# Angle signs by ScalarE, Fourier sums of two tiles and products of two blocks per VectorE instruction

## The chip, the cores and the metric

The kernel runs on one core of a Trainium2 chip. A core has TensorE (PE, with PEld for its weight loads), VectorE (DVE), ScalarE (ACT), GpSimd (POOL) and SyncE (SP), which here issues the DMAs. The metric is the device time of one execution in microseconds, taken as the median of several runs.

## The reference

Three stages follow each other: a gated linear recurrence, a Fourier mixing with a channel product, and a token and channel product.

```python
mag = np.sqrt(a_re * a_re + a_im * a_im)
scale = np.minimum(mag, 0.999) / (mag + 1e-06)
a_re_n, a_im_n = (a_re * scale, a_im * scale)
for t in range(S):                       # B, H, S, D = 4, 8, 768, 48
    new_re = ar * S_re - ai * S_im
    new_im = ar * S_im + ai * S_re
    S_re, S_im = (new_re + kv, new_im)   # kv = outer(k_t, v_t)
    y[:, :, t] = np.einsum('bhd,bhde->bhe', q[:, :, t], S_re)
...
X = np.fft.fft(np.fft.fft(x, axis=1), axis=2)
u = x + np.real(X)
un = (u - mean(u)) / np.sqrt(var(u) + 1e-06)
x = u + np.maximum(un @ w_ch1, 0.0) @ w_ch2
...
u = x + token product of x;  out = u + np.maximum(u @ w_ch1, 0.0) @ w_ch2
```

The complex gates are turned into a product of factors and a sum of angles along t: the running magnitude is a scan over logarithms, the running angle a scan over angles in turns. The angle of one gate is arctan of im / (mag + |re|), twice, with its sign and an offset of half a turn changed where re is negative. The queries and keys are multiplied by cosine and sine of the running angle and by the running magnitude, and what is left is attention within blocks of 128 steps and a state carried from block to block.

## The kernel before, in words

`recurrence_and_fourier` (line 41) holds the first two stages up to u; `channel_product` follows twice. Each engine has its instructions written out in its own order, and waits on semaphores with fixed counts.

**Parts and stages.** There are 24 blocks of 128 steps (six for each of four batches), one per iteration m = 0 to 23 of the loop in every engine's program; b, j = divmod(m, 6). The gates are worked on in nine parts: one of one block, one of two, seven of three. `stage_at` (line 72) places six stages of a part, 0 to 5, in the six iterations before its first block. Each part goes through: squares, `squared`, `magnitudes`, `logs` (with the scan of logarithms), `inverses`, `factors`, `ends`, `tangents`, `scaled`, then `arctangents` and `phases` (stage 3: multiplication by the sign, scan of the angles, rounding to the nearest turn), `sines` and `products` of two blocks (stage 4), `products` of the third (stage 5). The first three parts are done ahead of the loop or in its first iterations. Parts whose first block has j = 0 have their stage 3 in an iteration with j = 3, the others in one with j = 0.

**PE in iteration m.** Transposes of block m's keys (`turn_keys`, line 645; not for j = 5), outputs of block m - 1 from `pr` and the state (lines 669 and 671), mixed with the scores of block m (653), the state's update (682), then Fourier work of the batch before: for j = 1 the row of the middle and three width transforms (699, 714), and for j = 2 to 5 one or two of six inverse tiles (`sequence_transform`, lines 728 to 732), which leave in two PSUM banks `f_bank` by turns; last, the transposes of y of block m - 1 (`turn_y`, 690).

**DVE in iteration m.** `advance_state`, `add_transform` for tiles made in the iteration before, `fold_sequence` for j = 1, stages 3, 4 and 5, then `masked` (line 544: scores times mask into `pr`, without which PE can't compute block m's outputs), then stages 0, 1 and 2. DVE works strictly in this order.

**ACT in iteration m.** `arctangents`, `sines`, the copies of the turned keys, squares, magnitudes, inverses, factors, the copy of y to `y_sb`, for j = 1 the copies of the width transforms, and last the copy of turned y (line 360), which waits for the end of PE's iteration.

**SP** writes products of a block to DRAM and reads them back with the axes exchanged (`turn_over`), the same for the end factors (`turn_decay`), and loads the parts. It waits in its own order too; a wait holds back all that stands behind.

`least` (line 112) is the smallest end factor of all parts. Where it is under a floor, a slow exact path is taken behind this function.

Of the kernel before, what the change touches and what calls it, by code (L numbers as in the profile page):

```python
# [11 lines left out]
P = 128  # L12
# [28 lines left out]
def recurrence_and_fourier(nc, lay, c, u_out, w_raw, tok_raw, x_early, w2_early, w1_next, w2_next, steep):  # L41
    with ExitStack() as ctx:
# [31 lines left out]
        GA = 14  # L74
        GV = [12 + 5 * p.chunks for p in parts]
# [24 lines left out]
        dstage = sb("dstage", [P, 2, 3, 3])  # L100
# [11 lines left out]
        least, least_now, at_floor = sb("least", [P, 1]), sb("least_now", [P, 1]), sb("at_floor", [P, 1])  # L112

        bank = [ctx.enter_context(nc.psum_tensor(f"bank{i}", [P, 512], fp32)) for i in range(8)]
        tr_bank, sc_bank, st_bank, y_bank, f_bank = bank[0:2], bank[2:4], bank[4], bank[5], bank[6:8]
# [6 lines left out]
        consts_set, least_step = sem("consts_set"), sem("least_step")  # L122
# [22 lines left out]
        def transformed_at(j):  # L145
            return {2: [0], 3: [1, 2], 4: [3, 4], 5: [5]}.get(j, [])

        def added_at(m):
            b, j = divmod(m, NCH)
            n = b - 2 if j == 0 else b - 1  # L150
            return [(n, i) for i in {3: [0], 4: [1, 2], 5: [3, 4], 0: [5]}.get(j, []) if n >= 0]

        def products_done(p, i):
            return vec0[p.n] + 12 + 3 * p.chunks + 2 * i
# [5 lines left out]
        def _(sp):  # L160
# [44 lines left out]
            def turn_decay(p):  # L205
# [3 lines left out]
                for part in range(2):  # L209
                    sp.dma_start(lay["d_turn"][p.s, part].rearrange("g p t -> p g t"),  # L210
                                 dstage[:, p.s, :, :]).then_inc(d_out[p.s], 16)
# [28 lines left out]
            for m in range(NM):  # L240
# [8 lines left out]
                for n, i in added_at(m - 1):  # L249
                    store_u(n, i)  # L250
                if m % 3 == 1:
# [11 lines left out]
                if m == NM - 3:  # L263
# [6 lines left out]
                    for p in parts[-2:]:  # L270
                        sp.wait_ge(vec_step[p.s], vec0[p.n] + 9)
# [7 lines left out]
            for n, i in added_at(NM - 1):  # L279
                store_u(n, i)  # L280
            store_u(B - 2, 5)
# [7 lines left out]
        def _(act):  # L289
            A = nc.scalar.activation  # L290

            def squares(p):
                s, T = p.s, slice(0, p.T)
                act.wait_ge(gates_in[p.r], 32 * (p.round + 1))
                if p.turn:
                    act.wait_ge(vec_step[s], vec0[p.n - 2] + 9)
# [3 lines left out]
            def magnitudes(p):  # L300
# [27 lines left out]
            def arctangents(p):  # L328
                s, T = p.s, slice(0, p.T)
                act.wait_ge(vec_step[s], vec0[p.n] + 6)  # L330
                A(t3_b[s][:, :, T], t3_b[s][:, :, T], ACT.Arctan).then_inc(act_step[s], 1)

            def sines(p):
                s, T, n = p.s, slice(0, p.T), act0[p.n]
                re, im = re_b[p.r], im_b[p.r]
                act.wait_ge(vec_step[s], vec0[p.n] + 11 + 3 * p.chunks)
                A(re[:, :, T], t3_b[s][:, :, T], ACT.Abs).then_inc(act_step[s], 1)
                A(im[:, :, T], t3_b[s][:, :, T], ACT.Sin, scale=TURN).then_inc(act_step[s], 1)
                act.wait_ge(act_step[s], n + 12)
# [37 lines left out]
            act.wait_ge(consts_set, 2)  # L377
# [1078 lines left out]
```

## Time and profile before

| | us |
|---|---|
| median of 3 runs | 1140.12 |
| the runs | 1132.46, 1140.42, 1140.12 |
| the profiled execution | 1143.03 |
| its span | 1141.3 |
| PE, DVE, ACT busy | 1019.5, 538.2, 341.9 |
| last inverse tile of the recurrence part | ends near 427 |

The profiled execution is 2.9 us above the median, and 1.7 us lie outside its span. The page gives averages over a span of which the recurrence part is the first 430 us; the change lies in it, so windows and timelines of that stretch say more. PE's busy time hides its speed: the same matmul takes twice as long at the lower of its two clocks, and counts as busy for longer.

### The profile page before, as it was taken

The numbers are of one execution on the slowest core, as the hardware profiler recorded it, in microseconds if no ns is written. First come the engines' busy times: TensorE is split into PE (matmuls) and PEld (weight loads), VectorE is DVE, ScalarE is ACT, GpSimd is POOL, SyncE is SP. The second block draws the span as 40 slices with busy tenths as digits, with TensorE's granted clock in tenths as the row PEclk, the third lists the DMA queues.
The fourth block names the chain that finished last, engine by engine and source line by source line (L and its number), as shares of the span: only waits on it lengthen the run. The fifth ranks groups of instructions, "written<-read, shape, count | busy, mean of one in ns | idle before, by whom it ended". The sixth has DMA issues, their size and how long they took to land. (4 is left out here: it accounts for less than half of the span.)

```text
span 1141.3 us, 15470 instructions
## 1 busy us (share of the span) xinstructions
PE 1019.5 (89%) x6034; PEld 992.7 (87%) x6034; DVE 538.2 (47%) x1040; ACT 341.9 (30%) x515; POOL 29.4 (3%) x14
## 2 busy tenths in 40 slices
PE   0269999979979991999999999977999999999998
PEld 0269999969969971999999999977999999999998
DVE  6797786997962338342432332216323322331411
ACT  6654544745620104211122122115221220310310
POOL 0000000000000004000000000004000000000000
PEclk9999997979977985999999999998999999999999
DMA  4569776774657011712102102001000100100000
GB/s 150 167 170 285 211 219 174 232 221 139 195 158 257 29 35 52 263 43 73 38 14 83 41 21 63 21 24 42 15 8 24 46 14 21 41 21 14 7 21 21
DMA packets 96886, 104.77 MB, mean 92 GB/s; under 512 B 13121, under 2 KB 90433, under 8 KB 96834
## 3 DMA queue, kind: packets, MB, share of 16 engines
q1 hardware_dynamic: 96834, 104.07, 29.6%
q8 instruction: 34, 0.56, 0.2%
q14 instruction: 18, 0.15, 0.0%
HBM read 70.93 MB, written 33.11 MB: 91 GB/s over the span
## 5 line engine op out<-in xcount | busy, mean ns | idle before, releaser
L1111 ACT ACTIVATE hh<-mbank 128x384 fp32r<-128x384 f32 x192 | 94.5, 492 | 370.6 <-PE mbank L1295 370.6
L1204 DVE SCALAR_TENSOR_TENSOR hl<-mbank,hh 128x384 fp32r<-128x384 f32 x192 | 107.0, 558 | 200.7 <-ACT hh L1111 200.7
L1293 PE MATMUL mbank<-nTh,w1h 128*128 128x384 f32 x576 | 193.7, 336 | 0.7 <-DVE w1l L1226 0.7
L1294 PE MATMUL mbank<-nTl,w1h 128*128 128x384 f32 x576 | 193.2, 335 | 0.0
L1295 PE MATMUL mbank<-nTh,w1l 128*128 128x384 f32 x576 | 193.1, 335 | 0.0
L1293 PE MATMUL mbank<-w2h,hh 128*128 128x384 f32 x576 | 193.1, 335 | 0.0
L1295 PE MATMUL mbank<-w2h,hl 128*128 128x384 f32 x576 | 192.4, 334 | 0.0
L1294 PE MATMUL mbank<-w2l,hh 128*128 128x384 f32 x576 | 192.4, 334 | 0.0
L1293 PEld LDWEIGHTS mbank<-nTh,w1h 128*128 128x128 f32 x576 | 108.8, 189 | 1.4 <-issue 1.3
L1294 PEld LDWEIGHTS mbank<-nTl,w1h 128*128 128x128 f32 x576 | 108.7, 189 | 0.0
L1295 PEld LDWEIGHTS mbank<-nTh,w1l 128*128 128x128 f32 x576 | 108.7, 189 | 0.0
L1294 PEld LDWEIGHTS mbank<-w2l,hh 128*128 128x128 f32 x576 | 108.2, 188 | 0.0
L1293 PEld LDWEIGHTS mbank<-w2h,hh 128*128 128x128 f32 x576 | 108.2, 188 | 0.0
L1295 PEld LDWEIGHTS mbank<-w2h,hl 128*128 128x128 f32 x576 | 108.1, 188 | 0.0
L653 PE MATMUL bank<-qT,kT 96*128 96x128 f32 x384 | 99.9, 378 | 1.0 <-DMA qT<-q_turn 1.0
L669 PE MATMUL bank<-v_sb,pr 128*128 128x48 f32 x384 | 79.5, 300 | 21.4 <-DVE pr L544 21.4
L669 PEld LDWEIGHTS bank<-v_sb,pr 128*128 128x128 f32 x384 | 76.1, 248 | 22.0 <-DVE pr L544 22.0
L653 PEld LDWEIGHTS bank<-qT,kT 96*128 96x128 f32 x384 | 74.9, 259 | 1.3 <-issue 1.3
L671 PE MATMUL bank<-state,qT 96*128 96x48 f32 x320 | 72.9, 315 | 0.0
L1218 DVE TENSOR_TENSOR out_sb<-mbank,tok_raw 128x384 f32<-128x384 f32 x24 | 13.4, 557 | 125.1 <-PE mbank L1295 125.1
L645 PE MATMUL bank<-ident,kT 96*128 96x96 f32 x160 | 25.2, 297 | 51.1 <-DMA kT<-k_turn 47.9
L645 PEld LDWEIGHTS bank<-ident,kT 96*128 96x128 f32 x160 | 19.8, 172 | 54.9 <-issue 41.3
(149 smaller groups left out, 1308.5 us busy)
## 6 DMA issues: line engine op xcount, KB each, us to landing
kT<-k_turn SPq DMA_DIRECT2D x24, 384.0 KB, 3.5
qT<-q_turn SPq DMA_DIRECT2D x24, 384.0 KB, 4.5
q_turn<-w_raw SPq DMA_DIRECT2D x30, 192.0 KB, 4.5
k_turn<-t SPq DMA_DIRECT2D x24, 192.0 KB, 4.0
k_turn<-w_early SPq DMA_DIRECT2D x24, 192.0 KB, 4.4
u_scratch<-y_sb SPq DMA_DIRECT2D x24, 192.0 KB, 2.7
w_raw<-in_moe_w_ch SPq DMA_DIRECT2D x2, 2304.0 KB, 9.7
x_early<-u_scratch SPq DMA_DIRECT2D x4, 1152.0 KB, 9.8
```

The source lines that it names most:

```text
L645: turned = nc.tensor.transpose(tr_bank[n % 2][:, g * HD2:(g + 1) * HD2], kT[:, r, 4 * half + g, :], ident[0:HD2, 0:HD2])
L653: made = mm(sc_bank[h // 4][:, (h % 4) * P:(h % 4 + 1) * P], kT[:, r, h, :], qT[:, r, h, :], start=True, stop=True)
L669: made = mm(y_bank[:, cols], pr[:, h, :], v_sb[:, p.s, m - p.first, cols], start=True, stop=not later)
L671: made = mm(y_bank[:, cols], qT[:, m % RING, h, :], state[:, n % 3, cols], start=False, stop=True)
L1111: nc.scalar.activation(hh[:, m, :], mm_bank[(g * (KF + TPG) + m) % 2][:, 0:TG], ACT.Relu).then_inc(h_high, 1)
L1204: nc.vector.scalar_tensor_tensor(out=hl[:, m, :], in0=mm_bank[(g * (KF + TPG) + m) % 2][:, 0:TG], scalar=0.0, in1=hh[:, m, :].bitcast(fp32 ...
L1218: nc.vector.tensor_tensor(out_sb[:, i % 2, :], mm_bank[2 + t % 2][:, 0:DM], res[:, i, :], ALU.add).then_inc(out_ready, 1)
L1293: nc.tensor.matmul(out, lh, rh, start=(n == 0), stop=False)
L1294: nc.tensor.matmul(out, lh, rl, start=False, stop=False)
L1295: last = nc.tensor.matmul(out, ll, rh, start=False, stop=(n == len(pairs) - 1))
```

## The change

- The two comparisons of re with zero leave DVE. ACT computes Sign(3 re + 1e-20) into the buffer of im behind each arctangent, and from it the offset 0.25 - 0.25 sign into `t4`. `phases` multiplies by the sign, and its scan reads the offset from `t4`. `t4` had one use (|re|) and has two now; the first part uses its last third (`angles_room`).
- `magnitudes` waits for the last scan of the two parts before, where it waited for the sum with |re| of the part before.
- `products` works on pairs of blocks (`PAIRS`): the first two of a part in one instruction of 768 elements per partition, the third alone.
- The two banks of the inverse tiles are one tensor `f_pair`, and `add_transform` adds two tiles per instruction, except for the last batch. Inverse tiles are made at j = 2 (two), 3 (two), 5 (two), where it was 2 (one), 3 (two), 4 (two), 5 (one), and added at j = 3, 4 and 0 of the next batch.
- Each part has its own room in `dstage`, and the least end factor is found by one reduction behind the loop; `ends` is one copy and no longer waits for `d_out`.
- Counts of semaphores follow.

```diff
-            return {2: [0], 3: [1, 2], 4: [3, 4], 5: [5]}.get(j, [])
+            return {2: [0, 1], 3: [2, 3], 5: [4, 5]}.get(j, [])
...
-            return [(n, i) for i in {3: [0], 4: [1, 2], 5: [3, 4], 0: [5]}.get(j, []) if n >= 0]
+            return [(n, i) for i in {3: [0], 4: [2], 0: [4]}.get(j, []) if n >= 0]
...
-                if p.n:
-                    act.wait_ge(vec_step[1 - s], vec0[p.n - 1] + 3)
-                A(t4[:, :, T], re_b[p.r][:, :, T], ACT.Abs).then_inc(act_step[s], 1)
+                for o in parts[max(p.n - 2, 0):p.n] if p.n > 1 else []:
+                    act.wait_ge(vec_step[o.s], vec0[o.n] + 7 + 3 * o.chunks)
+                A(t4[:, :, angles_room(p)], re_b[p.r][:, :, T], ACT.Abs).then_inc(act_step[s], 1)
...
                 A(t3_b[s][:, :, T], t3_b[s][:, :, T], ACT.Arctan).then_inc(act_step[s], 1)
+                A(im_b[p.r][:, :, T], re_b[p.r][:, :, T], ACT.Sign, scale=3.0,
+                  bias=nearly_zero[:, 0:1]).then_inc(act_step[s], 1)
+                act.wait_ge(act_step[s], act0[p.n] + 12)
+                A(t4[:, :, angles_room(p)], im_b[p.r][:, :, T], ACT.Identity, scale=-0.25,
+                  bias=quarter[:, 0:1]).then_inc(act_step[s], 1)
...
-                if p.turn:
-                    dve.wait_ge(d_out[s], 32 * p.turn)
-                V.tensor_copy(dstage[:, s, :, 0:p.chunks], t2_b[s][:, :, CT - 1:p.T:CT]).then_inc(vec_step[s], 1)
-                dve.wait_ge(vec_step[s], vec0[p.n] + 5)
-                V.tensor_reduce(least_now[:, :], dstage[:, s, :, 0:p.chunks], mybir.AxisListType.XY,
-                                ALU.min).then_inc(least_step, 1)
-                dve.wait_ge(least_step, 2 * p.n + 1)
-                V.tensor_tensor(least[:, :], least[:, :], least_now[:, :], ALU.min).then_inc(least_step, 1)
+                V.tensor_copy(dstage[:, p.n, :, 0:p.chunks], t2_b[s][:, :, CT - 1:p.T:CT]).then_inc(vec_step[s], 1)
...
-                dve.wait_ge(vec_step[s], n + 6)
-                V.tensor_scalar(im[:, :, T], re[:, :, T], 0.0, -2.0 / PI, ALU.is_lt, ALU.mult).then_inc(vec_step[s], 1)
...
-                dve.wait_ge(act_step[s], act0[p.n] + 11)
-                dve.wait_ge(vec_step[s], n + 7)
-                V.scalar_tensor_tensor(out=t3_b[s][:, :, T], in0=im[:, :, T], scalar=1.0 / PI, in1=t3_b[s][:, :, T],
-                                       op0=ALU.add, op1=ALU.mult).then_inc(vec_step[s], 1)
-                dve.wait_ge(vec_step[s], n + 10)
-                V.tensor_scalar(im[:, :, T], re[:, :, T], 0.0, 0.5, ALU.is_lt, ALU.mult).then_inc(vec_step[s], 1)
+                dve.wait_ge(act_step[s], act0[p.n] + 13)
+                V.scalar_tensor_tensor(out=t3_b[s][:, :, T], in0=t3_b[s][:, :, T], scalar=1.0 / PI, in1=im[:, :, T],
+                                       op0=ALU.mult, op1=ALU.mult).then_inc(vec_step[s], 1)
...
-                for i in chunks:
-                    T = slice(i * CT, (i + 1) * CT)
+                for pair in chunks:
+                    i = pair.start
+                    T = slice(i * CT, pair.stop * CT)
...
-            def add_transform(b, i):
-                n = b * NT + i
-                x = y_sb[:, n % YR, :]
-                dve.wait_ge(b_made, n + 1)
-                cc, sn = f_bank[i % 2][:, 0:FH], f_bank[i % 2][:, FH:2 * FH]
+            def add_transform(b, i, tiles):
+                n, halves_done = b * NT + i, len(halves_added) + 1
+                halves_added.append(n)
+                x = y_sb[:, n % YR:n % YR + tiles, :]
+                dve.wait_ge(b_made, n + tiles)
+                f = f_pair[:, i % 2:i % 2 + tiles, :]
+                cc, sn = f[:, :, 0:FH], f[:, :, FH:2 * FH]
...
-            add_transform(B - 2, 5)
-            dve.wait_ge(least_step, 2 * len(parts))
+            add_transform(B - 2, 4, 2)
+            V.tensor_reduce(least[:, :], dstage[:, :, :, :], mybir.AxisListType.XYZ, ALU.min).then_inc(least_found, 1)
+            dve.wait_ge(least_found, 1)
...
                 if b:
-                    pe.wait_ge(b_added, b * NT - 1)
+                    pe.wait_ge(b_added, b * NT)
```

**Where instructions stand now.** On ACT, iteration 15 before (t_1 holds the tangent, then the arctangent of the part):

```order
L360 ACTIVATE yT<-bank 128x3x128 [waits folded,tr_made]
L331 ACTIVATE t_1<-t_1 128x1152 [waits vec_step_1]
L346 ACTIVATE kt<-bank 128x384 [waits tr_made] x2
L297 ACTIVATE x_early<-re 128x1152 [waits vec_step_0,gates_in_2]
L298 ACTIVATE tok_raw<-im 128x1152
L353 ACTIVATE y_sb<-bank 128x384 [waits u_stored_2,y_made]
```

and in the changed kernel, from the same copy of yT (t without a number is `t4`):

```order
L372 ACTIVATE yT<-bank 128x3x128 [waits folded,tr_made]
L338 ACTIVATE t_1<-t_1 128x1152 [waits vec_step_1]
L339 ACTIVATE w_raw<-w_raw,nearly_zero 128x1152
L342 ACTIVATE t<-w_raw,quarter 128x1152 [waits act_step_1]
L358 ACTIVATE kt<-bank 128x384 [waits tr_made] x2
L304 ACTIVATE x_early<-re 128x1152 [waits vec_step_0,gates_in_2]
```

Sign and Identity stand between the arctangent and the copy of the turned keys, kt.

On DVE, iteration 15 before, from `add_transform` to the first scan:

```order
L566 TENSOR_TENSOR y_sb<-y_sb,bank 128x193 [waits b_made]
L567 TENSOR_TENSOR y_sb<-y_sb,bank 128x191
L569 TENSOR_TENSOR y_sb<-y_sb,bank 128x193 [waits b_half]
L570 TENSOR_TENSOR y_sb<-y_sb,bank 128x191
L487 SCALAR_TENSOR_TENSOR t_1<-w_raw,t_1 128x1152 [waits vec_step_1,act_step_1]
L490 TENSOR_SCALAR w_raw<-w_raw 128x1152 [waits vec_step_1]
L499 SCALAR_TENSOR_TENSOR t_1<-t_1,w_raw 128x128 [waits vec_step_1]
```

and now:

```order
L573 TENSOR_TENSOR y_sb<-y_sb,f_pair 128x2x193 [waits b_made]
L574 TENSOR_TENSOR y_sb<-y_sb,f_pair 128x2x191
L576 TENSOR_TENSOR y_sb<-y_sb,f_pair 128x2x193 [waits b_half]
L577 TENSOR_TENSOR y_sb<-y_sb,f_pair 128x2x191
L489 SCALAR_TENSOR_TENSOR t_1<-t_1,w_raw 128x1152 [waits act_step_1]
L501 SCALAR_TENSOR_TENSOR t_1<-t_1,t 128x128 [waits vec_step_1]
```

Four instructions of two tiles stand where four of one tile stood, and the comparison ahead of the scan is gone; what `phases` waits for is ACT's count alone.

On PE, the end of iteration 14 (j = 2) before, from the state's update to `turn_y`:

```order
L682 MATMUL bank<-v_sb,kt 96x48 [waits st_free,tr_free,v_in_1]
L682 MATMUL bank<-v_sb,kt 96x48 x7
L728 MATMUL bank<-a_mid,tok_raw 128x193 [waits a_ready]
L730 MATMUL bank<-a_sb,cs 128x193 x3
L732 MATMUL bank<-a_sb,ss 128x193 x3
L690 MATMUL bank<-ident,y_sb 128x128 [waits tr_free,y_ready]
L690 MATMUL bank<-ident,y_sb 128x128 x2
```

and now (f_pair are the two banks of the inverse tiles):

```order
L691 MATMUL bank<-v_sb,kt 96x48 [waits st_free,tr_free,v_in_1]
L691 MATMUL bank<-v_sb,kt 96x48 x7
L735 MATMUL f_pair<-a_mid,tok_raw 128x193 [waits a_ready]
L737 MATMUL f_pair<-a_sb,cs 128x193 x3
L739 MATMUL f_pair<-a_sb,ss 128x193 x3
L735 MATMUL f_pair<-a_mid,tok_raw 128x193 [waits a_ready]
L737 MATMUL f_pair<-a_sb,cs 128x193 x3
L739 MATMUL f_pair<-a_sb,ss 128x193 x3
L699 MATMUL bank<-ident,y_sb 128x128 [waits tr_free,y_ready]
L699 MATMUL bank<-ident,y_sb 128x128 x2
```

A second inverse tile stands between the first and `turn_y`. In iteration 16 (j = 4) there is none now.

## Rows read from the trace of the kernel before

**Rows 1.** The page, part 1: engine, busy us (share of the span), instructions.

```profile
PE 1019.5 (89%) x6034; PEld 992.7 (87%) x6034; DVE 538.2 (47%) x1040; ACT 341.9 (30%) x515; POOL 29.4 (3%) x14
```

**Rows 2.** What PE waited for, 40 to 450 us: total us, times, longest us.

```profile
PE bank L669 <- DVE pr L544: 21.4, 3, 8.0
```

**Rows 3.** Timeline of PE: start us, us, line, op, operands, [idle before <-releaser].

```profile
68.04 1.51 PE L669 MATMUL bank<-v_sb,pr 128*128 128x48 f32 x6 [6.39 <-DVE pr L544]
...
135.83 1.54 PE L645 MATMUL bank<-ident,kT 96*128 96x96 f32 x8 [1.79 <-DMA kT<-k_turn]
...
239.04 1.51 PE L669 MATMUL bank<-v_sb,pr 128*128 128x48 f32 x6 [7.00 <-DVE pr L544]
...
321.60 1.51 PE L669 MATMUL bank<-v_sb,pr 128*128 128x48 f32 x6 [7.97 <-DVE pr L544]
```

**Rows 4.** Windows of 6 us, PE: length, busy (instructions), granted clock, DMA share, GB/s.

```profile
84.00:90.00 6.00, 6.00 (x30) 1.00 1.03 317
174.00:180.00 6.00, 6.00 (x32) 0.50 0.89 222
240.00:246.00 6.00, 6.00 (x29) 0.50 0.78 285
270.00:276.00 6.00, 6.00 (x59) 1.00 0.19 44
```

**Rows 5.** Timeline of PE: turn_y, which ends an iteration (8; 13, 14, 15; 20, 21).

```profile
186.47 0.85 PE L690 MATMUL bank<-ident,y_sb 128*128 128x128 f32 x3
...
257.53 0.49 PE L690 MATMUL bank<-ident,y_sb 128*128 128x128 f32 x3
...
268.42 0.49 PE L690 MATMUL bank<-ident,y_sb 128*128 128x128 f32 x3
...
281.94 0.49 PE L690 MATMUL bank<-ident,y_sb 128*128 128x128 f32 x3
...
350.67 0.49 PE L690 MATMUL bank<-ident,y_sb 128*128 128x128 f32 x3
...
372.27 0.49 PE L690 MATMUL bank<-ident,y_sb 128*128 128x128 f32 x3
```

**Rows 6.** Timeline of DVE: start of `phases` in iterations 9 and 15, second comparison.

```profile
188.93 1.36 DVE L487 SCALAR_TENSOR_TENSOR t<-im,t 128x1152 f32<-128x1152 f32 x1 [0.94 <-ACT t L331]
...
272.54 1.35 DVE L487 SCALAR_TENSOR_TENSOR t<-w_raw,t 128x1152 f32<-128x1152 f32 x1
...
273.92 0.76 DVE L490 TENSOR_SCALAR w_raw<-w_raw 128x1152 f32<-128x1152 f32 x1
```

**Rows 7.** Timeline of DVE: copy of the end factors, first multiplication of `tangents`.

```profile
304.78 0.16 DVE L459 COPY dstage<-tok_raw 128x9 f32<-128x9 f32 x1
...
305.25 1.35 DVE L470 TENSOR_TENSOR t<-im,t 128x1152 f32<-128x1152 f32 x1
```

**Rows 8.** Timeline of DVE: a 768-element product; then a pair's first, and what follows.

```profile
26.68 0.95 DVE L479 TENSOR_TENSOR w_early<-w_early,x_early 128x768 f32<-128x768 f32 x1
...
154.62 0.56 DVE L515 TENSOR_TENSOR t<-w_early,w_raw 128x384 f32<-128x384 f32 x1
...
158.74 1.28 DVE L544 TENSOR_TENSOR pr<-bank,mask 128x512 f32<-128x512 f32 x2
```

**Rows 9.** Timeline of DVE: first instruction of two tiles' sums, one after the other.

```profile
216.67 0.35 DVE L566 TENSOR_TENSOR y_sb<-y_sb,bank 128x193 f32<-128x193 f32 x1
...
217.84 0.35 DVE L566 TENSOR_TENSOR y_sb<-y_sb,bank 128x193 f32<-128x193 f32 x1
```

**Rows 10.** Timeline of ACT: copy of yT, arctangent, an operation with bias column.

```profile
268.95 0.49 ACT L360 ACTIVATE yT<-bank 128x384 f32<-128x384 f32 x1 [3.05 <-PE bank L690]
...
269.34 1.16 ACT L331 ACTIVATE t<-t 128x1152 f32<-128x1152 f32 x1
...
284.96 1.25 ACT L340 ACTIVATE w_raw<-w_raw,half_pi 128x1152 f32<-128x1152 f32 x1
```

More of the change, by code:

```diff
@@ L72, in recurrence_and_fourier @@
         stage_at = {(p.first - LEAD + k, k): p for p in parts[2:] for k in range(LEAD)}
-        GA = 14
-        GV = [12 + 5 * p.chunks for p in parts]
+        PAIRS = [[range(i, min(i + 2, p.chunks)) for i in range(0, p.chunks, 2)] for p in parts]
+        GA = 16
+        GV = [10 + 3 * p.chunks + 2 * len(PAIRS[p.n]) for p in parts]
         act0 = [GA * p.turn for p in parts]
@@ L150, in added_at, with angles_room @@
             n = b - 2 if j == 0 else b - 1
-            return [(n, i) for i in {3: [0], 4: [1, 2], 5: [3, 4], 0: [5]}.get(j, []) if n >= 0]
+            return [(n, i) for i in {3: [0], 4: [2], 0: [4]}.get(j, []) if n >= 0]
         def products_done(p, i):
-            return vec0[p.n] + 12 + 3 * p.chunks + 2 * i
+            return vec0[p.n] + 10 + 3 * p.chunks + 2 * (i // 2)
+        def angles_room(p):
+            return slice(2 * CT, 3 * CT) if p.n == 0 else slice(0, p.T)
         head_view = lambda ap: ap.rearrange("p (h d) -> p h d", h=H)
@@ L210, in turn_decay @@
                     sp.dma_start(lay["d_turn"][p.s, part].rearrange("g p t -> p g t"),
-                                 dstage[:, p.s, :, :]).then_inc(d_out[p.s], 16)
+                                 dstage[:, p.n, :, :]).then_inc(d_out[p.s], 16)
                 if p.turn:
@@ L250, in _ @@
                     store_u(n, i)
+                    store_u(n, i + 1)
                 if m % 3 == 1:
@@ L278, in _ @@
                     sp.dma_start(w2_early, w2_next.rearrange("(k p) n -> p k n", p=P)).then_inc(w_fetched, 16)
-            for n, i in added_at(NM - 1):
-                store_u(n, i)
-            store_u(B - 2, 5)
+            for i in (4, 5):
+                store_u(B - 2, i)
             for i in range(NT):
@@ L498, in phases @@
                             start = carry[:, 1 - s, g:g + 1] if p.j0 else 0.0
-                        last = V.tensor_tensor_scan(t3_b[s][:, g, T], t3_b[s][:, g, T], im[:, g, T], start, ALU.add, ALU.add)
+                        last = V.tensor_tensor_scan(t3_b[s][:, g, T], t3_b[s][:, g, T], t4[:, g, offset], start, ALU.add, ALU.add)
                     last.then_inc(vec_step[s], 1)
-                    dve.wait_ge(vec_step[s], n + 12 + 3 * i)
+                    dve.wait_ge(vec_step[s], n + 10 + 3 * i)
                     V.tensor_scalar(re[:, :, T], t3_b[s][:, :, T], ROUND, ROUND, ALU.add, ALU.subtract).then_inc(vec_step[s], 1)
-                    dve.wait_ge(vec_step[s], n + 13 + 3 * i)
+                    dve.wait_ge(vec_step[s], n + 11 + 3 * i)
                     V.tensor_tensor(t3_b[s][:, :, T], t3_b[s][:, :, T], re[:, :, T], ALU.subtract).then_inc(vec_step[s], 1)
-                dve.wait_ge(vec_step[s], n + 11 + 3 * p.chunks)
+                dve.wait_ge(vec_step[s], n + 9 + 3 * p.chunks)
                 V.tensor_copy(carry[:, s, :], t3_b[s][:, :, p.T - 1]).then_inc(vec_step[s], 1)
@@ L591, in _ @@
             phases(p1)
-            products(p0, range(1))
+            products(p0, PAIRS[0])
             squared(p2)
-            products(p1, range(2))
+            products(p1, PAIRS[1])
             logs(p2)
@@ L610, in _ @@
                 if (m, 4) in stage_at:
-                    products(stage_at[m, 4], range(2))
+                    products(stage_at[m, 4], PAIRS[stage_at[m, 4].n][0:1])
                 if (m, 5) in stage_at:
-                    products(stage_at[m, 5], [2])
+                    products(stage_at[m, 5], PAIRS[stage_at[m, 5].n][1:2])
                 masked(m)
```

51 lines of the change are left out of this document (28 added, 23 removed).

## The prediction

> **What bounds the kernel now.** The page comes first. TensorE (PE) is busy for most of the span, VectorE (DVE) for about half [rows 1]. The change touches only the recurrence part, which ends with the last inverse tile near 427 us; the 710 us behind it are the two channel products, whose instructions, order and buffers the diff leaves alone. I price those at nothing, and what they cost comes back unchanged.
>
> Inside the recurrence the list of what PE waited for names one DVE instruction, the masked scores `pr` [rows 2], and the timeline of PE puts that wait at three places: the start (output of block 0 at 68.04), block 12 at 239.04 after 7.00 us, block 18 at 321.60 after 7.97 us [rows 3]. The fourth row there is a wait of 1.79 us for a DMA. Between these places PE doesn't wait, so DVE time that is saved there buys nothing unless it brings one of the waits forward.
>
> The second thing is PE's own speed. Two windows of 6 us with PE busy throughout hold 30 and 59 matmuls [rows 4]: the first stretch (up to about 162 us) runs at 1.2 GHz, although its record says 1.00, and most of what comes behind at 2.4. The record reads 0.50 after each long wait for `pr`, and also at 174 to 180 us, where PE was busy without a gap [rows 4]. The fall in iteration 21 (350.67 to 372.27, 21.6 us) costs 8.1 us against the same work in iteration 15 (268.42 to 281.94, 13.5 us) [rows 5].
>
> The Trainium skill (TensorE: Matmul & The Clock Gate, Part 1) says that the clock is low by default, rises with sustained activity and falls after idleness. The falls behind the two waits agree; the busy window at 84 us and the fall at 174 us don't, and the measurement decides. By the page alone the clock would fall at those two waits and nowhere else, the sum below would be the same, and the two cases of a fall fewer or more would have no chance.
>
> **Removed from DVE.** Per part of three blocks: the two comparisons with zero, 0.76 us each and about 0.04 of gap [rows 6], 0.8 and 0.7 net; the reduction and the minimum behind the copy of the end factors, which leave 0.2 of the 0.47 us between the copy and the next row [rows 7], 0.3 saved. The products of a pair: eight instructions take 4.12 us, start to start [rows 8]; four of 768 elements at 0.95 or a little less [rows 8] take 3.6 to 3.8; I take 0.5 saved, between 0.3 and 0.6. Fourier sums: one tile takes 1.17 us [rows 9], two in one call four instructions of 386 elements, priced by the 384-wide rows at 4.12 / 8 = 0.52 each, so 2.0 instead of 2.34. The single reduction at the end and the missing wait on `d_out` in `ends` lie under the outputs of block 23: nothing on the path; if that cover were gone, 0.2 us.
>
> **Added to ScalarE (ACT).** Sign and Identity behind each arctangent, both with a bias column: 1.25 us by the row of that form, against 1.16 without one [rows 10]. Started back to back they lengthen 1.16 us to about 3.5, so +2.35 us per part, and the first DVE instruction of `phases` now waits for the last of them. Behind them on ACT stand the copies of the turned keys, which PE's state update needs 6 us later: covered.
>
> **Moved.** Inverse tile 1 goes from iteration j = 3 to j = 2, tile 3 from 4 to 3, tile 4 from 4 to 5. PE's sum of work is the same. But at j = 3 DVE adds tiles 0 and 1 in one call, ahead of `phases`, so both must be made: one tile more of PE time, about 2.7 us at 2.4 GHz (10.9 us for iteration 14 with one tile, 13.5 for iteration 15 with two [rows 5]), up to twice that at 1.2. The same tile holds back the copy of yT on ACT, and so the arctangent. Past SP's queue nothing new is moved: the two stores of u behind a pair go out together.
>
> **Stretch B, iterations 14 to 18.** Now yT is copied at 268.95 and the arctangent starts at 269.34 [rows 10], ending at 270.5; `phases` starts at 272.54 [rows 6], so ACT had 2.0 us in hand. With the tile and the two operations it starts 2.7 + 2.35 - 2.0 = 3.0 us later. From there to 321.60 [rows 3] DVE has hardly a gap, and its work shrinks by 0.8 + 0.8 (second comparison, twice), 0.7 (first, once), 0.3 (ends), 0.5 (products), and sums 5 x 1.17 - 2 x 2.0 = 1.9: 5.0 in all. The logarithms of iteration 17 have 1 us in hand against ACT now; I charge 0.5 for their wait. Result: 3.0 - 5.0 + 0.5 = **-1.5 us**. PE's own work up to there is the same, less a small wait of 1 us that now comes for block 16 or so, so the long wait ends near 5.5 us, and the clock falls as before.
>
> **Stretch A, iterations 8 to 12.** Here `phases` started at 188.93 [rows 6] with nothing in hand: it was ACT that released it. The second tile is made behind 186.47 [rows 5], where the clock is just rising: 2.9 us. So 2.9 + 2.35 = 5.2 later, 5.0 less work, **+0.2 us** at 239.04 [rows 3].
>
> **Start.** The comparison saved ahead of the first `masked` would bring 68.04 forward by 1.3 us, 0.8 of it that instruction and 0.5 from the first products, which start the chain of DMAs. But PE then meets the wait at 135.83 [rows 3] on a DMA of that chain, which moves only by the 0.5: the rest is given back. **-0.5 us** (0 to -1.3).
>
> **Last batch and end.** In iterations 19 to 23 DVE has no `phases` left and PE doesn't wait: 0. The six single sums at the end keep their form: 0.
>
> **Sum:** -1.5 + 0.2 - 0.5 = -1.8 us. The profiled execution took 1143.0; the median shown is 1140.1, 2.9 lower, so 1138.3, and I say 1138. The unknown costs reach from -5 (no lateness on ACT in B, 1.3 at the start) to +3 (second tile at 1.2 GHz, 0.6 us each of further waits).
>
> **The rivals.**
>
> *All of the saving arrives (0.08).* If the second tile and the two ACT operations came in time, as they would if `phases` were not held at j = 3, both stretches would end 5.0 earlier, the waits would shrink to 2 and 3 us, and PE might keep 2.4 GHz. Taking the slow stretch behind each as two windows of 6 us like 240 to 246 [rows 4], worth half of 12: 1140.1 - 0.5 - 2 x 5.0 - 2 x 6 = 1118. For it: DVE is full there. Against it: 188.93 was released by ACT already.
>
> *One fall of the clock fewer (0.17).* The three times shown are 1132.5, 1140.4, 1140.1; one lies 8 us lower, as much as the fall in iteration 21 costs. The busy stretches in which the clock fell (iterations 8 and 21) look like others in which it didn't (14, 15). With two tiles in a row at j = 2 the light stretch ahead of iteration 21 is broken by more dense work. 1138 - 8 = 1130. That both are missing: 0.03, 1122.
>
> *Slower: the clock falls in the light iteration (0.12).* At j = 4 PE now has no tile at all. The light stretch from the tiles of iteration 21 to those of 23 is 10.9 - 2.7 = 8.2 us plus some 5 of the next (the same work less the keys' transposes, an estimate), 13 to 14 at 2.4 GHz, where a tile stood between before. A fall some 4 us into it, as at 174 us, leaves about 10 us of work at half speed and none of DVE's slack to hide it, because PE is the bound in the last batch: +10, so 1148 when it comes in addition to the others. It decides if the record falls to 0.50 in iteration 22. In iterations 10 and 16 the same fall would mostly eat PE's long wait.
>
> *The change does not do what it says:* if the merged instructions cost as much as those they replace, B loses 2.4 of its 5.0 and A as well, PE's long waits keep their length, and the time is 1140 to 1143, inside the forecast's own spread.
>
> **How the numbers follow.** Forecast 0.60, the rivals as given, both falls missing 0.03 among them. The forecast alone spans 1133 to 1143. 1127 to 1148 takes in the cases of one fall less and one more and leaves out 1118, 1122 and tails, less than 2 in 10. About 1% is what a measurement of this kernel can tell from no change: faster than 1128.7 are the first rival (0.08), both falls missing (0.03) and a third of the 1130 case (0.06): 0.17. Slower than 1151.5 needs two more falls: 0.04. Within: 0.79.
>
> **What would show it.** In the new profile: rows for Sign and Identity near 1.2 us; `phases` of iterations 9 and 15 released by ACT Identity, and starting 4 to 5 and 3 us later; PE waiting 5 to 6.5 us for `pr` of blocks 12 and 18; iteration 10, 16, 22 with no tile near 8.2 us; DVE's total some 25 us lower, ACT's some 20 higher; PE's wait for kT(6) longer by about 0.8. Waits for `pr` under 3 us, or a granted clock that stays at 1.00 behind them, would make it wrong on the fast side; 0.50 in iteration 22 on the slow side.

## The result, and the profile after

| | before | after |
|---|---|---|
| median, us (runs) | 1139.31 (8) | 1147.65 (8) |
| lowest and highest run, us | 1132.46, 1145.16 | 1145.76, 1150.01 |
| ratio, 95% interval | | 1.0091, 1.0061 to 1.0121 |
| profiled execution, us | 1143.03 | 1149.2 |
| last `turn_y` starts at, us | 398.73 | 403.82 |
| profiled execution less that start | 744.3 | 745.4 |

The change made the kernel 0.9% slower; forecast was 0.2% faster. (The ratio is the one on record, with its interval; that of the two medians is 1.0073.) The last row says that all but 1 us of the difference of the two profiled executions lies ahead of the last `turn_y`, so in the recurrence, as the prediction assumed.

The page, busy time by engine (the answer to [rows 1]):

```profile
PE 1021.5 (89%) x6034; PEld 995.0 (87%) x6034; DVE 517.5 (45%) x938; ACT 361.7 (32%) x533; POOL 29.4 (3%) x14
```

DVE lost 20.7 us (25 were forecast), ACT gained 19.8 (20). The 25 were too much by the prediction's own prices: over nine parts and nine pairs of tiles they make about 12 for the comparisons, 4 for the products, 3 for the sums and 3 for the end factors, 22 in all. So the instructions do about what they were priced at. What PE waited for, with total, times and longest, the answer to [rows 2]:

```profile
PE bank L654 <- DMA kT<-k_turn: 49.7, 4, 41.3
PE bank L678 <- DVE pr L547: 14.8, 3, 5.8
PE bank L699 <- ACT y_sb L365: 6.6, 3, 3.0
```

The wait for `pr` shrank from 21.4 us to 14.8. The third line is what changed most: three times, in `turn_y`, PE waits for ScalarE's copy of y, where it was once for 0.6 us before. The timeline of PE at the waits (idle time in brackets), the answer to [rows 3, 5]; L699 is `turn_y`:

```profile
138.83 1.54 PE L654 MATMUL bank<-ident,kT 96*128 96x96 f32 x8 [4.93 <-DMA kT<-k_turn]
187.99 0.49 PE L699 MATMUL bank<-ident,y_sb 128*128 128x128 f32 x3
201.51 0.49 PE L699 MATMUL bank<-ident,y_sb 128*128 128x128 f32 x3
212.83 0.90 PE L699 MATMUL bank<-ident,y_sb 128*128 128x128 f32 x3 [3.00 <-ACT y_sb L365]
231.30 0.49 PE L699 MATMUL bank<-ident,y_sb 128*128 128x128 f32 x3
239.46 0.51 PE L699 MATMUL bank<-ident,y_sb 128*128 128x128 f32 x3
245.61 1.51 PE L678 MATMUL bank<-v_sb,pr 128*128 128x48 f32 x6 [4.51 <-DVE pr L547]
334.45 1.52 PE L678 MATMUL bank<-v_sb,pr 128*128 128x48 f32 x6 [4.51 <-DVE pr L547]
380.01 0.49 PE L699 MATMUL bank<-ident,y_sb 128*128 128x128 f32 x3
388.18 0.51 PE L699 MATMUL bank<-ident,y_sb 128*128 128x128 f32 x3
399.24 0.49 PE L699 MATMUL bank<-ident,y_sb 128*128 128x128 f32 x3
```

From one `turn_y` to the next is one iteration. Iteration 10 (201.51 to 212.83) holds no tile and took 11.3 us, 3.00 of them the wait. Iteration 11 took 18.5; iteration 23, with the same two tiles, took 11.1 (388.18 to 399.24). Windows of PE (PE busy and matmuls, granted clock, DMA share, GB/s) say why:

```profile
204.00:210.00 6.00, 5.84 (x56) 1.00 0.28 91
210.00:216.00 6.00, 3.17 (x16) 0.61 0.82 207
216.00:222.00 6.00, 6.00 (x30) 0.50 0.72 205
...
378.00:384.00 6.00, 5.75 (x48) 1.00 0.47 164
384.00:390.00 6.00, 6.00 (x60) 1.00 0.09 34
```

Behind the new wait the granted clock is 0.50, which is 1.2 GHz, and in iteration 22 (380.01 to 388.18), the same PE work without a wait, it stays at 1.00 (the window 384 to 390 reaches into iteration 23). Why y came late is in ACT's timeline of iteration 10:

```profile
206.55 1.28 ACT L384 ACT_TABLE_LOAD   x1
207.85 1.16 ACT L310 ACTIVATE x_early<-x_early 128x1152 f32<-128x1152 f32 x1
209.04 1.25 ACT L312 ACTIVATE tok_raw<-x_early,ln_eps 128x1152 f32<-128x1152 f32 x1
210.21 1.15 ACT L316 ACTIVATE t<-x_early 128x1152 f32<-128x1152 f32 x1
211.26 1.15 ACT L319 ACTIVATE t<-w_raw 128x1152 f32<-128x1152 f32 x1
212.31 0.47 ACT L365 ACTIVATE y_sb<-bank 128x384 f32<-128x384 f32 x1
```

A table load and the four operations of `magnitudes` stand ahead of the copy of y (L365) in each iteration of stage 1. The kernel before has them in the same order. There the copy was done before PE came to `turn_y`; its two rows:

```profile
211.16 0.47 ACT L353 ACTIVATE y_sb<-bank 128x384 f32<-128x384 f32 x1
213.87 0.49 PE L690 MATMUL bank<-ident,y_sb 128*128 128x128 f32 x3
```

What hid them were the two inverse tiles (5.4 us) that PE made in iteration j = 4 ahead of `turn_y`; the change took both away.

### The profile page after: what moved, and what is told of

The parts are those of the page before. It is cut to its first block and busy times, and to the rows that moved or that the text cites. A ratio compares the mean times of both kernels' runs of the same rounds, so it can differ in the third digit from the quotient of the medians.

```text
span 1147.4 us, 15375 instructions
## 1 busy us (share of the span) xinstructions
PE 1021.5 (89%) x6034; PEld 995.0 (87%) x6034; DVE 517.5 (45%) x938; ACT 361.7 (32%) x533; POOL 29.4 (3%) x14
## 5 line engine op out<-in xcount | busy, mean ns | idle before, releaser
L678 PE MATMUL bank<-v_sb,pr 128*128 128x48 f32 x384 | 81.2, 305 | 14.8 <-DVE pr L547 14.8
L654 PEld LDWEIGHTS bank<-ident,kT 96*128 96x128 f32 x160 | 19.3, 169 | 57.1 <-issue 41.3
```

The lines of the kernel that those rows point to most:

```text
L654: turned = nc.tensor.transpose(tr_bank[n % 2][:, g * HD2:(g + 1) * HD2], kT[:, r, 4 * half + g, :], ident[0:HD2, 0:HD2])
L678: made = mm(y_bank[:, cols], pr[:, h, :], v_sb[:, p.s, m - p.first, cols], start=True, stop=not later)
```

## The experiments

Ratios are to the kernel before on the same chip; the chips of two experiments can differ, so ratios are compared and not medians. The diffs are against the changed kernel unless the text says otherwise, `...` marks what is left out, and changed counts of semaphores are left out everywhere. Iteration lengths are differences of starts of `turn_y`, from one profiled execution of each kernel.

### Which part costs

**e3_single_tiles**: the Fourier part undone.

```diff
-            return {2: [0, 1], 3: [2, 3], 5: [4, 5]}.get(j, [])
+            return {2: [0], 3: [1, 2], 4: [3, 4], 5: [5]}.get(j, [])
...
-                    add_transform(n, i, 2)
+                    add_transform(n, i, 1)
...
```

> The changed kernel with its Fourier part undone: the table of tiles and one tile per DVE instruction as before; signs on ACT, paired products and the single reduction stay. W and L: the falls in 10 and 16 go, the one in iteration 8 or 21 may come back: 1136 to 1142. A: 1146 to 1149.

**e4_signs_dve**: the comparisons back on DVE.

```diff
-                A(im_b[p.r][:, :, T], re_b[p.r][:, :, T], ACT.Sign, ...)
...
-                A(t4[:, :, angles_room(p)], im_b[p.r][:, :, T], ACT.Identity, ...)
...
+                V.tensor_scalar(im[:, :, T], re[:, :, T], 0.0, -2.0 / PI, ALU.is_lt, ALU.mult).then_inc(vec_step[s], 1)
...
+                V.tensor_scalar(im[:, :, T], re[:, :, T], 0.0, 0.5, ALU.is_lt, ALU.mult).then_inc(vec_step[s], 1)
```

> The changed kernel with its signs undone: both comparisons back on DVE, no Sign and Identity on ACT; paired tiles with their new table and paired products stay. W and L: the wait for y_sb and the falls stay, DVE has 1.6 us more work per part: 1146 to 1152. A: the lateness of phases goes, 1137 to 1141.

**e5_fourier_alone**: e4, and the products block by block.

```diff
-        PAIRS = [[range(i, min(i + 2, p.chunks)) for i in range(0, p.chunks, 2)] for p in parts]
+        PAIRS = [[range(i, i + 1) for i in range(p.chunks)] for p in parts]
```

> The kernel before with the new places of the inverse tiles, the sums of two tiles per instruction and the single reduction of the end factors; signs and offset by VectorE and products block by block, as before. Theory (the new places of the tiles carry the loss): ratio to before 1.006 to 1.014, PE waiting near 3 us for y_sb in iterations 10 and 16. Rival (the loss needs the parts together): 0.998 to 1.004.

**e8_two_sums**: tiles made and added at the new places, but by two calls.

```diff
-                    add_transform(n, i, 2)
+                    add_transform(n, i, 1)
+                    add_transform(n, i + 1, 1)
```

> The changed kernel, tiles made and added at the same places, but each pair added by two calls of one tile (eight instructions of 193 or 191 elements in place of four of 386 or 382). Theory (the places carry the loss, not the merged instruction): within 2 us of the changed kernel, ratio to before 1.007 to 1.013, DVE busy some 2 us more. Rival (the merged instruction holds DVE back): ratio 0.998 to 1.003.

| kernel | median, us | ratio, 95% interval |
|---|---|---|
| e3_single_tiles | 1136.18 | 0.9978, 0.9948 to 1.0008 |
| e4_signs_dve | 1148.41 | 1.0119, 1.0070 to 1.0169 |
| e5_fourier_alone | 1143.97 | 1.0091, 1.0054 to 1.0127 |
| e8_two_sums | 1144.45 | 1.0078, 1.0049 to 1.0106 |

Without the Fourier part the loss is gone; alone it is there in full. All four lie with the theory that was put down for them. PE's waits for `y_sb` are three and 6.6 us in sum in e4, e5 and e8, as in the changed kernel, and one of 0.6 us in e3. So it is the place of the tiles and not the merged instruction. Signs on ACT cost nothing that can be seen.

### The wait for y, or the place without a tile

**e1_y_early** moves ACT's copy of y between the two exponentials of the magnitudes, **e7_y_first** ahead of both, in all iterations that have stage 1 (j = 1 and 4).

```diff
                 A(t2_b[s][:, :, T], t1_b[s][:, :, T], ACT.Exp, scale=-0.5, ...)
+                if m_now:
+                    evacuate_y(m_now - 1)
```

> The changed kernel, with one thing moved on ACT: in an iteration with stage 1 (m = 4, 10, 16) the copy of y to y_sb stands between the first and second Exp of magnitudes, not behind |re|. Theory W (wait): at j = 4 PE has no inverse tile, meets turn_y at once and waits 3.0 us for y_sb, which ACT copies behind magnitudes; this idle time makes the clock fall in iterations 10 and 16. Then the wait shrinks to 1 us or less, both falls go, and the time is 1134 to 1140. Theory L (light work): the clock falls because the iteration has no dense matmuls, wait or not. Then the falls stay and the time is 1145 to 1149. Theory A (Sign and Identity make DVE late): 1146 to 1149.

> The changed kernel, with ScalarE's copy of y moved ahead of both exponentials of the magnitudes, right behind their logarithm, so that PE should not wait for y_sb at all in iterations 4, 10 and 16 (0.9 us were left when the copy stood one instruction later). Theory W (the wait drops the clock in iterations 10 and 16): no fall there, ratio to before 0.985 to 0.993. Theory L (the iteration without a tile is too light, whatever the wait): the clock falls in iterations 10 and 16 all the same, ratio 0.998 to 1.004.

**e2_tile_in_4** puts a tile back to j = 4, so that the second pair is added at j = 5.

```diff
-            return {2: [0, 1], 3: [2, 3], 5: [4, 5]}.get(j, [])
+            return {2: [0, 1], 3: [2], 4: [3], 5: [4, 5]}.get(j, [])
```

> The changed kernel, with inverse tile 3 made in iterations with j = 4 and the pair 2, 3 added at j = 5: tiles 0,1 / 2 / 3 / 4,5 for j = 2, 3, 4, 5. Still two tiles per DVE instruction. Theories W and L both expect the wait for y_sb and the falls in iterations 10 and 16 gone: 1134 to 1140. Theory A expects no change: 1146 to 1149.

**e9_filler** fills j = 4 with the matmuls of a tile made for nothing, into the bank that `turn_y` overwrites; the output is the same. **e16_filler_10_16** has it in iterations 10 and 16 alone.

```diff
+                if m >= NCH and (m + 1) % NCH == 4:      # e16: if m + 1 in (10, 16)
+                    out = tr_bank[n % 2]
+                    mm(out[:, 0:FH], alt[:, 0:P], a_mid[:, :], start=True, stop=False)
+                    ...
                 pe.wait_ge(y_ready, m + 1)
```

> The changed kernel, with the matmuls of one inverse tile made once more and for nothing in iterations 10, 16 and 22, ahead of turn_y, into the bank that turn_y then overwrites: 2.7 us of useless PE work where PE waited 3.0 us for y_sb. Theory (the place without a tile costs by the wait and by the clock that falls behind it): the wait becomes 0.3 us, no fall behind it in iterations 10 and 16, 7.4 us each less and 2.7 more in iteration 22: ratio to before 0.996 to 1.001. Rival (the wait only costs its own length): the filler buys nothing, ratio 1.009 to 1.014.

> The changed kernel with the useless tile in iterations 10 and 16 alone. In e9_filler (10, 16 and 22) the last batch took 78.2 us from turn_y of block 17 to that of block 23, with a fall of the clock near 380 us, in the changed kernel 75.5 without one. Theory (it fell because of the filler's place, and 2.7 us of filler there pay nothing): 3 us less than e9_filler, ratio to before 0.993 to 0.997. Rival (a fall comes in the last batch anyway): as e9_filler or above, 0.997 to 1.001.

| kernel | median, us | ratio, 95% interval | wait for y in iterations 10 and 16, us each | iteration 10 / 11, us |
|---|---|---|---|---|
| before | | | none | 13.5 / 8.4 (2 tiles / 1) |
| after | 1147.65 | 1.0091, 1.0061 to 1.0121 | 3.0 | 11.3 / 18.5 (0 / 2) |
| e1_y_early | 1136.93 | 1.0016, 0.9991 to 1.0042 | 0.9 | 9.2 / 19.3 |
| e7_y_first | 1139.01 | 1.0029, 0.9999 to 1.0059 | none | 8.2 / 17.2 |
| e2_tile_in_4 | 1144.05 | 1.0100, 1.0065 to 1.0135 | none | 19.2 / 11.1 |
| e9_filler | 1133.56 | 0.9986, 0.9962 to 1.0010 | 0.3 | 11.3 / 11.1 |
| e16_filler_10_16 | 1129.59 | 0.9945, 0.9924 to 0.9967 | 0.3 | 11.3 / 11.1 |

e9_filler is the clearest: PE does 2.7 us of useless work where it had waited 3.0, iteration 10 takes as long as in the changed kernel, and iteration 11 falls from 18.5 to 11.1 us. Its windows over the same stretch:

```profile
204.00:210.00 6.00, 5.68 (x48) 1.00 0.62 184
210.00:216.00 6.00, 6.00 (x37) 1.00 0.84 235
216.00:222.00 6.00, 5.75 (x53) 1.00 0.93 276
```

Since the useless work takes as long as the wait did, what the filler gains is the clock: e16_filler_10_16 is 1.5% under the changed kernel by ratio (0.9945 to 1.0091, 17 us). In the profiled executions iterations 7 to 18 took 15.1 us less (160.2 to 175.3), of which 13.9 are the falls behind iterations 10 and 16; the rival, that the wait costs its own length only, is out. DMA traffic is no rival either: in these windows of e9_filler its share is 0.84 and 0.93 with the clock at 1.00, in the changed kernel 0.72 with the clock at 0.50.

e7_y_first was meant to leave no wait. Its PE timeline shows that DVE supplied another, for the scores of block 10, and its windows that the clock fell behind it:

```profile
206.76 0.51 PE L701 MATMUL bank<-ident,y_sb 128*128 128x128 f32 x3
208.31 0.42 PE L680 MATMUL bank<-v_sb,pr 128*128 128x48 f32 x2 [1.04 <-DVE pr L549]
```

```profile
204.00:210.00 6.00, 4.96 (x48) 1.00 0.42 121
210.00:216.00 6.00, 6.00 (x36) 0.62 0.94 270
```

So W and L (the theories of e1_y_early and e7_y_first: the wait, or the light iteration as such) were not told apart by this run, whose ratio lies in the range of L: here the iteration without a tile was followed by a wait of 1.04 us, in e1_y_early it ended in one of 0.89 us, and the clock fell behind both.

```profile
204.30 0.55 PE L701 MATMUL bank<-ident,y_sb 128*128 128x128 f32 x3 [0.89 <-ACT y_sb L367]
```

The profiles taken together speak for W. Iteration 22 had no tile and no wait in eight of them (after, e1, e4, e5, e7, e8, e14, e16), and took 8.2 us at 1.00 in all eight; iteration 12 of the kernel before (222.24 to 230.40, no tile, DMA share 0.79) ran at 1.00 as well. Behind an unfilled wait of 0.89 to 3.0 us in iterations 10 or 16, or right behind them, the clock fell in all fourteen cases (two each in after, e1, e2, e4, e5, e7 and e8). With a filler and a wait of 0.32 us left it fell in none of twelve (e9, e10, e12, e13, e14, e16). A kernel with light iterations 10 and 16 and no wait at all was not made.

Copying y earlier (e1) still bought 0.75% by ratio, in the middle of what W forecast, but not by what W said: the two waits are 2.1 us shorter each, and the falls are still there. In the profiled executions iterations 7 to 18 took 6.3 us less (169.1 to 175.3).

e2_tile_in_4 missed both W and L, which had 1134 to 1140. The wait for y is gone, but iteration 9 has a tile less in front of it, PE came to `pr` sooner and waited for it five times instead of three (18.1 us in all): 1.67 and 1.68 us at the start of iterations 10 and 16, and the clock fell behind both. The gap had only moved, and the ratio is the changed kernel's. In its profile the clock also fell in iteration 22, which has a tile there and no gap over 0.25 us, and took 16.9 us instead of 10.8:

```profile
197.75 0.42 PE L678 MATMUL bank<-v_sb,pr 128*128 128x48 f32 x2 [1.67 <-DVE pr L547]
```

```profile
372.00:378.00 6.00, 6.00 (x40) 0.68 0.11 38
378.00:384.00 6.00, 6.00 (x29) 0.50 0.00 0
```

So a gap in iterations 10 and 16 was followed by a fall each time, with or without a tile behind it; but falls also come without a gap.

In e16_filler_10_16 the last batch took 75.3 us from `turn_y` of block 17 to that of block 23, the changed kernel 75.5, e9_filler 78.2: the tile in iteration 22 was 2.7 us for nothing.

### ScalarE's two operations a stage earlier

From iteration 3 on every `phases` of the changed kernel waits for ACT's Identity (L342), 1.1 to 2.3 us; two rows of DVE's timeline:

```profile
231.50 0.56 DVE L573 TENSOR_TENSOR y_sb<-y_sb,f_pair 128x386 f32<-128x386 f32 x1 [2.92 <-PE f_pair L739]
235.83 1.36 DVE L489 SCALAR_TENSOR_TENSOR t<-t,w_raw 128x1152 f32<-128x1152 f32 x1 [2.26 <-ACT t L342]
```

**e10_filler_signs_early** (on e9_filler) and **e11_single_early** (on e3_single_tiles) put Sign and Identity into the iteration before, ahead of the copy of yT.

```diff
+                if (m, 2) in stage_at:
+                    signs(stage_at[m, 2])
                 if m:
                     y_turned(m - 1)
```

> The changed kernel with the useless tile in iterations 10, 16, 22 (as e9_filler) and with Sign and Identity moved from behind the arctangent to the iteration before it, ahead of ScalarE's copy of yT, where ScalarE waited some 3 us for PE. If the two operations held phases back (VectorE waited 2.26 us for Identity at every phase), phases start about 2 us earlier, PE waits about 2.5 us instead of 4.5 for pr of blocks 12 and 18, and the ratio to before is 0.993 to 0.997 against 0.9986 for the filler alone. Rival (the pair of sums, held by the second tile, hides them): no difference, 0.997 to 1.001.

> Tiles and single sums as in the kernel before, no filler; signs by ScalarE but an iteration early, products in pairs, single reduction. Against e3_single_tiles (0.9978) phases start up to 2 us earlier and the waits for pr shrink to about 2.5 us. Theory: ratio 0.992 to 0.998. Rival (the clock's falls decide, and they stay as many): 0.996 to 1.001.

Measured: 1137.67 us, 1.0015 (0.9989 to 1.0040), and 1142.31 us, 1.0089 (1.0052 to 1.0126). e10_filler_signs_early lies just above its rival's range (no gain), e11_single_early above both of its theories and 1.1% above e3_single_tiles. In e11_single_early DVE no longer waits 2.26 us at `phases`, and PE's waits for `pr` of blocks 12 and 18 are gone, but ACT now stands waiting for `tangents` ahead of its copy of yT, which PE needs for the next transposes. ACT and PE in iterations 17 and 18:

```profile
306.91 1.26 ACT L338 ACTIVATE im<-re,nearly_zero 128x1152 f32<-128x1152 f32 x1 [2.62 <-DVE t L483]
308.20 1.26 ACT L341 ACTIVATE t<-im,quarter 128x1152 f32<-128x1152 f32 x1
309.36 0.47 ACT L375 ACTIVATE yT<-bank 128x384 f32<-128x384 f32 x1
```

```profile
309.88 0.90 PE L662 MATMUL bank<-ident,kT 96*128 96x96 f32 x4 [3.60 <-ACT yT L375]
```

A wait of 4.5 us became one of 3.6 us a block earlier, and the clock fell behind that one: iteration 18 took 17.9 us (305.46 to 323.36) against 8.2. In e10_filler_signs_early the wait for yT at these places is 0.70 us; the clock stayed up behind the first and fell behind the second (iteration 18 took 12.7 us). In e13_all below, with the same two waits, it stayed up behind both. In all three kernels with early signs iteration 3 took 16.3 us, in e3_single_tiles and e9_filler 14.9.

### Filling the waits for pr

**e12_filler_pr** adds 3.8 us of useless matmuls ahead of the two long waits for `pr` to e9_filler, **e13_all** the earlier signs to that, **e14_filler_mid** has e12's fillers without that of iteration 22, **e15_before_filler_pr** puts 6.4 us there in the kernel before.

```diff
-                pe.wait_ge(sc_free, 2 * (m + 1))
...
                     pe.wait_ge(y_ready, m)
+                if before_wait:
+                    before_wait()      # matmuls of one and a half tiles into y_bank, m = 13 and 19
+                pe.wait_ge(sc_free, 2 * (m + 1))
```

> e9_filler with 3.8 us of useless matmuls more, ahead of PE's wait for pr of blocks 12 and 18, written to the bank of y that the outputs then overwrite. The waits for pr (4.5 us) should become under 1 us with no later end, since DVE sets it. Theory (a gap or light stretch is what the clock falls behind): no fall behind blocks 12 and 18, about 6 us each less: ratio to before 0.986 to 0.992. Rival (the clock falls there whatever fills the gap): 0.997 to 1.002.

> e12_filler_pr with Sign and Identity early as in e10. With phases 2 us earlier the 3.8 us of filler overshoot the wait for pr by up to 1.5 us each. Theory: as e12 or up to 2 us less, ratio 0.984 to 0.992. Rival (overshoot eats it): e12 or above.

> e12_filler_pr without the useless tile in iteration 22. Theory: no fall in iterations 10, 16, behind 12, 18 nor in the last batch, ratio 0.988 to 0.993 (the fall near 180 us stays). Rival (a fall comes in the last batch anyway): 0.993 to 0.997.

> The kernel before, with 6.4 us of useless matmuls ahead of PE's waits of 7.0 and 8.0 us for pr of blocks 12 and 18. Theory (the clock falls behind the gap, some 6 us each): ratio 0.988 to 0.993, the waits under 2 us. Rival (that fall costs nothing, since DVE sets the next wait): 0.997 to 1.002. If it comes out at or below e14_filler_mid, the change is worth nothing at a held clock either; its own sum said 1.8 us.

| kernel | median, us | range, us | ratio, 95% interval |
|---|---|---|---|
| e12_filler_pr | 1131.09 | 1123.68 to 1136.40 | 0.9939, 0.9907 to 0.9970 |
| e13_all | 1132.61 | 1123.61 to 1143.07 | 0.9978, 0.9943 to 1.0012 |
| e14_filler_mid | 1121.80 | 1121.02 to 1132.47 | 0.9871, 0.9835 to 0.9906 |
| e15_before_filler_pr | 1131.68 | 1123.30 to 1146.69 | 0.9926, 0.9899 to 0.9953 |

Fillers buy time at both kinds of place, but not each fall. e15_before_filler_pr has the ratio of its theory, e14_filler_mid lies just under its own (0.988 to 0.993), and e12_filler_pr missed it: 0.9939 against 0.986 to 0.992, about half the gain. None has the ratio of its rival, that a fall comes or costs nothing whatever fills the gap; only the upper end of e12's interval reaches it. e13_all lies with its rival and adds nothing to e12, as after e10. The best is the changed kernel with four fillers: by its six runs 1.3% faster than the kernel before, 2.2% than the changed one. e15 shows that the kernel before can be had 0.7% faster by the same means. Between the two lie 0.55% (0.9926 less 0.9871, some 6 us), where my sum for the change had 1.8 us. The two intervals just overlap, the fillers are not the same (e14 has those of iterations 10 and 16 as well), and the clock fell in both profiles, so what the change is worth with the clock held up is not settled.

In the profiled run of e12_filler_pr, the waits for `pr` are 0.86 us and the clock stays up behind both; the windows are those behind blocks 12 and 18 (the answer to the 0.50 window in [rows 4]):

```profile
240.00:246.00 6.00, 5.14 (x34) 1.00 0.44 126
246.00:252.00 6.00, 6.00 (x52) 1.00 1.04 368
...
324.00:330.00 6.00, 6.00 (x49) 1.00 0.33 99
```

It isn't so each time. In the profiled run of e15_before_filler_pr, with filled waits of 1.62 us left, the clock stayed up behind block 12 (236 us) and fell behind block 18 (313 us):

```profile
312.00:318.00 6.00, 4.62 (x25) 0.68 0.14 52
318.00:324.00 6.00, 6.00 (x31) 0.50 0.79 203
```

The profiled run of e14_filler_mid is the slowest of its six (1132.47 us; four of them lie at 1121.0 to 1122.2), and there the clock fell behind both filled waits (0.86 us left, as in e12), and in iteration 14, where PE had no gap over 0.31 us:

```profile
234.00:240.00 6.00, 6.00 (x39) 0.60 1.02 342
...
252.00:258.00 6.00, 6.00 (x33) 0.52 0.87 256
258.00:264.00 6.00, 6.00 (x25) 0.50 0.50 130
```

## Why the prediction was wrong, point by point

**The step that failed** is "PE's own work up to there is the same, less a small wait of 1 us that now comes for block 16 or so". PE's own work was the same, but the two tiles of j = 4 had been the cover of ACT's copy of y. I priced what the tiles hold back when they arrive (the sums, yT, the arctangent) and never asked what they had hidden where they stood. The wait was 3.0 us in iterations 10 and 16, and the clock fell behind it.

**The second** is "In iterations 10 and 16 the same fall would mostly eat PE's long wait." The mechanism was on the list, as the slower rival, but put into iteration 22, where it did not come. In iterations 11 and 17 it cost 18.5 - 11.1 = 7.4 and 17.6 - 11.1 = 6.5 us, and the long waits shrank by only 2.5 and 3.5. DVE was not full there: it waited 2.92 us for the late tiles at 231.50 and 2.26 for Identity at 235.83, as shown above. What delays PE in these iterations delays DVE's inputs, so the slack was not there to be eaten. Stretch B shows it whole. DVE's window from `phases` of iteration 15 to the long wait's end, before and after, and the two largest of its waits after, beside those for Identity:

```profile
272.50:321.60 49.10, 47.85 (x101) 0.96 0.58 170
```

```profile
282.20:334.40 52.20, 43.33 (x79) 0.87 0.55 159
```

```profile
311.58 0.69 DVE L547 TENSOR_TENSOR pr<-bank,mask 128x512 f32<-128x512 f32 x1 [1.97 <-PE bank L680]
320.33 0.56 DVE L573 TENSOR_TENSOR y_sb<-y_sb,f_pair 128x386 f32<-128x386 f32 x1 [2.84 <-PE f_pair L739]
```

DVE's work shrank by 4.5 us (5.0 forecast), and its idle time grew from 1.3 to 8.9.

In the terms of the sum, start of `turn_y` to end of the wait for `pr`: B, from iteration 13 to block 18, took 64.1 us before and 70.3 after, +6.2 where -1.5 was forecast; A, from iteration 7 to block 12, 69.4 and 71.2, +1.8 where +0.2 was; the part up to iteration 6, +3.0 where the start had -0.5; the last batch from iteration 19 on, -8.1 where it had 0, by the fall that stayed away in iteration 21.

The measured 1147.65 us lies inside the stated range (1127 to 1148), next to the 1148 of the slower rival. That is luck: the rival had one fall, in iteration 22, and what came were two waits and two falls elsewhere, while two other falls stayed away.

Profiled execution against profiled execution, after less before: waits for y +6.0, the falls behind them +13.9, long iterations 13 and 19 (waits for `pr` and what follows) -5.6, the falls of iterations 8 and 21 missing -14.0, iteration 7 +1.8, the part up to iteration 6 +3.0, behind the recurrence +1.1: +6.2 of 6.2. By the medians it is 8.3.

The other points:
- Sign 1.24 us and Identity 1.26 by their groups' means (1.25 forecast); four sums of a pair take 2.08 us start to end (2.0).
- `phases` of the part with block 15 starts 18.1 us behind `turn_y` of block 12, 15.0 before: 3.1 later, 3.0 forecast. Released by Identity, as said. In iteration 9 it starts at 192.53 us, 3.6 later (4 to 5 were forecast), of which 1.5 had come about by `turn_y` of iteration 8 (187.99 against 186.47).
- PE's waits for `pr` of blocks 12 and 18 were 4.51 us, under the 5 to 6.5 forecast. That is on the fast side, and didn't help.
- Iteration 22 took 8.17 us (8.2 forecast) at a clock of 1.00: the slower rival as written was wrong.
- The clock did stay up in iterations 8 and 21 of the profiled run, the rival of one fall fewer, even twice; it had not been seen that two others would replace them. But these falls in busy stretches come and go: iteration 8 took 21.7 us in the profiled runs of e5_fourier_alone and of e12_filler_pr, 13.6 in those of e9_filler and e14_filler_mid, with the tiles in the same places. I can't name a cause.
- The wait for kT(6) grew by 3.1 us, not 0.8, but it was 0.7 to 2.4 us in e1, e5, e7 and e8, none in e9 and 5.1 us in e12, all with the tiles in the places of the changed kernel: it scatters from kernel to kernel, and 3.0 us of the profiled difference come with it.

## What to carry to other kernels

Before moving work on the engine that sets the time, list what it hides where it stands: the copy that another engine makes behind a long run of its own work will be uncovered. Where that engine's granted clock falls behind a wait, as here, price an uncovered wait by the wait and the slow stretch behind it, and look for cheap fillers before looking for saved instructions: here 13 us of useless matmuls made the changed kernel 2.2% faster, while 18 us less of VectorE time, with the tiles in their old places (e3_single_tiles), bought nothing that can be told from no change, and 21 us less, with the tiles moved, came with a loss of 0.9%. Moving an operation to where its engine idles is free only if it has its inputs by then, and if nothing behind it on the queue is awaited.

## What the runs showed of the hardware

Behind those of 0.89 to 1.04 us (e1_y_early, e7_y_first) it cost 5.1 to 8.2 us, against the 11.1 us of the same iteration with the clock up. Waits of 0.32 us with a filler ahead of them were followed by a fall in none of twelve; waits of 0.70 us for yT in one of four (e10_filler_signs_early, e13_all).
- With a filler ahead of the long waits for `pr` the clock stayed up in five of eight cases: both in e13_all (no wait over 0.35 us left) and in e12_filler_pr (0.86 us left), none in e14_filler_mid (0.86 us), one in e15_before_filler_pr (1.62 us).
- The clock also fell with PE busy and no gap over 0.31 us (e14_filler_mid at 252 us, the kernel before at 174 us, e2_tile_in_4 near 374 us), by some 6 to 8 us each time, and not at the same places in the profiles of the kernels. The runs of a kernel can lie in groups, as many us apart: e14_filler_mid at 1121.0 to 1122.2 with a mean granted clock of 0.973 to 0.977, 1128.2 with 0.968, and 1132.5 with 0.964.
- Matmuls that nobody reads made the kernel 1.5% faster (e16_filler_10_16 against the changed kernel, by ratio to before).
